# Attention stage: softmax sums after the value products, one reciprocal a head, maxima placed before them

## What is computed

```
mask = q_bucket[:, :, :, None] == k_bucket[:, :, None, :]     # hash of 6 sign bits of q @ proj, k @ proj
scores = scale * np.matmul(q, k.transpose(0, 1, 3, 2))
scores = np.where(mask, scores, -1e9)
scores = scores - np.max(scores, axis=-1, keepdims=True)
attn = np.exp(scores)
attn = attn / (np.sum(attn, axis=-1, keepdims=True) + 1e-09)
attn_out = np.matmul(attn, v)
```

## Time and profile before

| | us |
|---|---|
| median of 3 runs | 670.48 |
| lowest and highest | 669.12, 671.76 |
| the profiled execution | 669.12 |
| its span | 667.0 |

### The profile page before, as it was taken

How to read it: one execution, slowest core, us unless ns; L and a number is a source line. 1 busy time by engine, 2 the same in 40 slices (tenths; PEclk the granted TensorE clock), 3 DMA queues, 4 the chain that set the end, 5 groups by cost and what they waited for, 6 DMA issues and landing times.

```text
span 667.0 us, 9761 instructions
## 1 busy us (share of the span) xinstructions
PE 584.1 (88%) x2886; PEld 437.3 (66%) x2887; DVE 402.7 (60%) x557; ACT 258.7 (39%) x403; POOL 268.8 (40%) x188
## 2 busy tenths in 40 slices
PE   3889999999999979999999996108999999999994
PEld 1566556556566447888888874007887878788773
DVE  3659888888899546556656662724266455556511
ACT  1255454546554522222222243124255364464410
POOL 4378879888887832322332235530000000100101
PEclk9999999999999998999999997558999999999997
DMA  6789578696571011000000003277146645755400
GB/s 188 168 227 242 155 212 213 158 261 171 124 199 29 12 59 68 1 1 0 0 0 0 0 1 126 91 258 259 56 167 209 240 159 179 270 163 180 151 4 30
DMA packets 39266, 83.90 MB, mean 126 GB/s; under 512 B 7485, under 2 KB 10429, under 8 KB 39232
## 3 DMA queue, kind: packets, MB, share of 16 engines
q1 hardware_dynamic: 31376, 71.04, 36.0%
q10 hardware_dynamic: 5616, 6.12, 3.6%
q0 software_dynamic: 2240, 6.31, 2.4%
HBM read 52.09 MB, written 12.35 MB: 97 GB/s over the span
## 4 chain that ended last, share of the span: by engine, by line
PE 75%; ACT 5%; issue 5%; DVE 4%; DMA 4%; POOL 3%; SPq 2%; ACTq 2%; DVEq 0%; POOLq 0%
PE PS L504 9%; PE PS L492 5%; PE PS L662 5%; PE PS L664 4%; PE PS L663 4%; PE PS L472 4%; PE PS L493 4%; PE PS L535 4%; PE PS L643 3%; PE PS L537 3%; PE PS L536 3%; PE PS L644 3%; PE PS L645 3%; PE PS L576 3%; PE PS L578 3%
## 5 line engine op out<-in xcount | busy, mean ns | idle before, releaser
L1033 ACT ACTIVATE at_PT<-PS 128x384 f32<-128x384 f32 x192 | 84.5, 491 | 100.5 <-PE PS L493 99.8
L1248 POOL TENSOR_TENSOR at_acc<-at_acc,at_PT 128x768 f32<-128x768 f32 x64 | 108.0, 1687 | 8.7 <-ACT at_PT L1033 2.8
L958 DVE TENSOR_TENSOR at_W<-at_raw,at_W 128x2048 f32 (+1 forms) x30 | 67.8, 2289 | 70.8 <-ACT at_W L1103 68.2
L728 DVE TENSOR_REDUCE sb_nm<-PS 128x1 f32<-128x768 f32 x96 | 90.2, 955 | 23.1 <-PE PS L472 18.5
L1324 POOL DMA_INDIRECT out<-at_yb,sb_to x16 | 15.8, 986 | 204.9 <-DVE at_yb L970 204.9
L1103 ACT ACTIVATE at_W<-at_raw 128x2048 f32 (+1 forms) x32 | 60.2, 1910 | 60.3 <-issue 34.5
L492 PE MATMUL PS<-at_A,at_B 102*128 102x384 f32 x192 | 75.1, 391 | 7.6 <-ACT at_PT L1033 7.6
L504 PE MATMUL PS<-at_PT,at_V 128*64 128x385 f32 x384 | 68.4, 489 | 2.4 <-ACT at_PT L1033 2.4
L493 PE MATMUL PS<-at_A,at_B 128*128 128x384 f32 x192 | 66.9, 349 | 0.0
L1279 POOL TENSOR_TENSOR at_cn<-at_eb,sb_mv 128x1024 f32<-128x1024 f32 x12 | 22.7, 1896 | 108.0 <-DVE sb_mv L784 108.0
L472 PE MATMUL PS<-at_B,at_A 76*128 76x384 f32 x192 | 57.9, 390 | 6.7 <-DMA at_B<-at_HB 4.7
(11 more groups left out here) (154 smaller groups left out, 1099.5 us busy)
## 6 DMA issues: line engine op xcount, KB each, us to landing
at_raw<-w SPq DMA_DIRECT2D x32, 1024.0 KB, 5.4
at_A<-at_H SPq DMA_DIRECT2D x32, 192.0 KB, 2.7
at_B<-at_H SPq DMA_DIRECT2D x28, 192.0 KB, 3.7
rows_by_expert<-at_empty SPq DMA_DIRECT2D x19, 257.0 KB, 5.3
at_XS<-rows_by_expert ACTq DMA_DIRECT2D x17, 256.0 KB, 2.7
at_stg<-w_solu SPq DMA_DIRECT2D x16, 256.0 KB, 4.1
at_V<-vP SPq DMA_DIRECT2D x16, 192.0 KB, 3.9
at_Re<-qT SPq DMA_DIRECT2D x4, 384.0 KB, 5.0
```

What stands on the lines that cost most here:

```text
L728: dve.tensor_reduce(nm[:, col:col + 1], slot(h, j), AX.XY, ALU.max, negate=True).then_inc(s_nm, 1)
L1033: fn(PT[:, kt, g, 0:HALF], PS[:, STB + g, 0:HALF], ACT.Exp, scale=SCALE).then_inc(s_exp, 1)
L1248: pool.tensor_tensor(total, PT[:, 0, :, 0:HALF] if kt == 1 else total, PT[:, kt, :, 0:HALF], ALU.add).then_inc(s_acc, 1)
```

## The change

PE's order at kt = 2 becomes `turn_maxima(h+1)`, `values(h-1, (3,4,5))`, `sums(h-1)` (before: sums, values, turn). The turn waits for `s_rec` (bank RB read by the sums of two heads before) and for `s_bits`; the sums wait for `s_mc` (the maxima placed), since they share bank RB. At the end `values(15)` stands ahead of `sums(15)`. On DVE `place_maxima(h+1)` moves ahead of the work on head h - 1; the three reciprocals of 128 columns become one of 384, directly behind the denominators; the copy of the epsilon column (L759) moves ahead of them; and `maximum(h+2, 1)` comes behind the whole reciprocal. The wait of `attended` on `s_pv` goes, since `s_rb` now implies it. SP's `load_v(h)` waits for `s_rb >= h - 1`, the sums of head h - 2, in place of `s_pv`. The counts of `s_rec` change from six to three a head.

```diff
@@ -388,7 +388,7 @@
                     fill_2(sp, h, n)
 
             def load_v(h):
-                wait(sp, s_pv, 2 * h - 2)
+                wait(sp, s_rb, h - 1)
                 sp.dma_start(V[h % 2], vP[h:h + 1].rearrange("o p (k d) -> p (o k) d", k=KT)).then_inc(ld_v[h % 2], 16)
 
             def load_w(m):
@@ -475,7 +475,6 @@
 
             def turn_maxima(h):
                 pe.wait_ge(s_mm, h + 1)
-                wait(pe, s_rec, 6 * (h - 1) - 5)
                 m = pe.transpose(PS[0:TILES, RB, 0:P], mm_[:, h % 2 * TILES:(h % 2 + 1) * TILES], ident)
                 m.then_inc(s_mt, 1)
 
@@ -508,8 +507,7 @@
             def sums(h):
 
                 pe.wait_ge(s_acc, (KT - 1) * (h + 1))
-                pe.wait_ge(s_bits, min(PAIRS, 2 + h // 2 + 1))
-                pe.wait_ge(s_mc, min(HEADS, h + 2))
+                wait(pe, s_rec, 3 * h - 1)
                 for g in range(2):
                     m = mm(PS[g * D:(g + 1) * D, RB, 0:HALF], cst[:, C_ONE:C_ONE + D],
                            acc[h % 2][:, g * HALF:(g + 1) * HALF], start=True, stop=True)
@@ -545,18 +543,22 @@
                         leading(*ahead)
                     products(h, kt)
                     if kt == 2:
+                        if h + 1 < HEADS:
+                            wait(pe, s_rec, 3 * h - 4)
+                            pe.wait_ge(s_bits, min(PAIRS, 2 + (h + 1) // 2))
+                            turn_maxima(h + 1)
                         if h > 0:
+                            values(h - 1, (3, 4, 5))
+                            if h + 1 < HEADS:
+                                pe.wait_ge(s_mc, h + 2)
                             sums(h - 1)
-                            values(h - 1, (3, 4, 5))
-                        if h + 1 < HEADS:
-                            turn_maxima(h + 1)
                 values(h, (0, 1, 2))
                 if h % 2 == 0 and h // 2 + 2 < PAIRS:
-                    pe.wait_ge(s_mc, h + 2)
+                    wait(pe, s_rec, 3 * h - 1)
                     hashes(h // 2 + 2, RB)
             hidden(0, 0, 0, True)
+            values(HEADS - 1, (3, 4, 5))
             sums(HEADS - 1)
-            values(HEADS - 1, (3, 4, 5))
             hidden(0, 0, 1, True)
 
 
@@ -743,27 +745,24 @@
                                   ident[0:TILES, 0:TILES].unsqueeze(2).broadcast_to([TILES, TILES, P]),
                                   ALU.mult).then_inc(s_mc, 1)
 
-            def sums_out(h):
+            def inverse(h):
+
                 dve.wait_ge(s_rb, h + 1)
+                dve.tensor_copy(mu[:, h % 2:h % 2 + 1], PS[:, PVB, HALF:HALF + 1]).then_inc(s_rec, 1)
                 dve.tensor_scalar(rec, PS[:, RB, 0:HALF], EPS, None, ALU.add).then_inc(s_rec, 1)
-
-            def inverse(h, n):
-
-                dve.wait_ge(s_rec, 6 * h + 1)
-                dve.reciprocal(rec[:, n * P:(n + 1) * P], rec[:, n * P:(n + 1) * P]).then_inc(s_rec, 1)
+                dve.wait_ge(s_rec, 3 * h + 2)
+                dve.reciprocal(rec, rec).then_inc(s_rec, 1)
 
             def attended(h):
 
                 p, c = h // 2, h % 2
-                dve.wait_ge(s_pv, 2 * h + 2)
-                dve.tensor_copy(mu[:, c:c + 1], PS[:, PVB, HALF:HALF + 1]).then_inc(s_rec, 1)
-                dve.wait_ge(s_rec, 6 * h + 5)
+                dve.wait_ge(s_rec, 3 * h + 3)
                 for g in range(2):
                     mine = slice(g * D, (g + 1) * D)
                     m = dve.scalar_tensor_tensor(
                         out=xT[c * D:(c + 1) * D, p * S + g * HALF:p * S + (g + 1) * HALF], in0=PS[mine, PVB, 0:HALF],
                         scalar=mu[mine, c:c + 1], in1=rec[mine, :], op0=ALU.add, op1=ALU.mult)
-                    m.then_inc(s_rec if g == 0 else s_fin, 1)
+                m.then_inc(s_fin, 1)
 
             def soft(n, b, first):
                 h2 = PS[:, 2 * b:2 * b + 2, :]
@@ -809,23 +808,18 @@
                     hash_bits(h // 2 + 2, RB)
                 if h + 2 < HEADS:
                     maximum(h + 2, 0)
+                if h + 1 < HEADS:
+                    place_maxima(h + 1)
                 if h > 0:
-                    sums_out(h - 1)
-                    inverse(h - 1, 0)
-                    inverse(h - 1, 1)
+                    inverse(h - 1)
                 if h + 2 < HEADS:
                     maximum(h + 2, 1)
                 if h > 0:
-                    inverse(h - 1, 2)
                     attended(h - 1)
-                if h + 1 < HEADS:
-                    place_maxima(h + 1)
                 if h + 2 < HEADS:
                     maximum(h + 2, 2)
                     maximum(h + 2, 3)
-            sums_out(HEADS - 1)
-            for n in range(3):
-                inverse(HEADS - 1, n)
+            inverse(HEADS - 1)
             attended(HEADS - 1)
             soft(0, 0, True)
 
```

## The result

The changed kernel takes 713.26 us in the median of 4 runs (712.05 to 714.27), the kernel before 670.26 in the same comparison. Over all 15 of its runs on record the changed kernel lies between 705.62 and 714.27, with a median of 710.96; the ratio of 1.0609 (95% interval 1.0567 to 1.0651) belongs to these 15, while the two medians of 4 would give 1.064. I had forecast 702.0 (690 to 709). The direction was right, the size too small by 9 to 11 us. The profiled execution of the changed kernel took 709.7 us; its span is 707.6 against 667.0. Nearly all of the 40.6 lies in attention: DVE's L771, the first instruction behind it, starts at 286.71, where it started at 246.43, 40.3 later.

What follows compares the result with a forecast made beforehand. PE taken as the bound, with DVE's chain from sums to values without slack; 30.0 + 1.94 + 1.94 - 0.5 - 0.5 - 0.4 = +32.5 us on 669.1 gives 701.6; predicted 702.0, range 690 to 709.

Steps and rivals of the forecast that it cites:

- DVE's chain without slack: From the end of sums to values(8), DVE's chain takes 5.82 us and PE's work there arrives together with it.
- Sums come 2.14 later: At kt = 2, turn (0.20) and values (1.94) ahead of sums make their end 2.14 us later in each head.
- T to values 5.84: T is the end of sums at kt = 2; in the changed kernel the next values start 5.84 us after it.
- leading(h+2, 3) ends last, by 0.2: On PE, its wait for maximum(h+2,1), 2.3 us, rather than the wait for s_fin, sets when values start, by 0.2.
- No new wait in turn, hashes, SP: The new waits of turn and hashes on PE, and of SP's V loads, would cost nothing.
- Tail: Passes 14 and 15 give back 0.5 us each, values ahead add 1.94 twice, the last chain gives back 0.4.
- The clock: Rival, 5%: PE's 2.3 us pause in every head drops its clock, adding 32 us, for 734 us.
- The rival's price: Loss at the low clock behind each of 14 pauses: 11 matmuls x 0.21 = 2.3 us.
- its sign, L472 at double length behind the pause: Sign of the falling clock: L472 on PE behind the pause runs at double length for more than one instruction.

Runs made afterwards that it cites:

- chain_longer: Kernel before with one more unused reduction ahead of maximum(h+2,1) on DVE in the passes of heads 1 to 13; 683.07 us, ratio 1.0193.
- one_reciprocal: Kernel before with one reciprocal of 384 columns for three of 128, maximum(h+2,1) behind it, PE's order kept; 668.06 us, ratio 0.9948.
- maximum_between: Changed kernel with three reciprocals of 128 columns again and maximum(h+2,1) between the second and third; 703.94 us, ratio 1.0488.
- pause_filled: Changed kernel with 12 small unused matmuls ahead of leading(h+2,3) in the passes of heads 1 to 13; 699.84 us, ratio 1.0436.
- pause_half: Changed kernel with 5 small unused matmuls ahead of leading(h+2,3) in the passes of heads 1 to 13; 706.74 us, ratio 1.054.

## Why the prediction fell short

**DVE's chain without slack: right.** In chain_longer a head grows by the whole 0.87 that was added. The profile's name for the releaser, ACT, was wrong, and the working from the code's own wait was right.

**Sums come 2.14 later: right.** In the chain of waits of the changed kernel, same pass:

```profile
158.84 0.11 PE PS L478
158.95 2.09 PE PS L503 x12
161.04 0.67 PE PS L512 x4
```

These three are 2.87 us, where the sums alone were 0.80: +2.07.

**T to values 5.84: too long.** It is 167.18 - 161.68 = 5.50. The gap of 0.13 ahead of the maximum was PE's doing and vanished, the maximum itself is 0.90 and not 0.96, PE restarts 0.05 behind it and not 0.15, and the copy takes 0.08 of the chain and not 0.14. The reciprocal was priced right: its row is 2.55 long, but the maximum starts 164.86 - 162.39 = 2.47 behind its start. A head at full clock grows by 1.62 to 1.71 (14.08 against 12.46, 15.99 against 14.28) and not by 2.14; 12 of them by 20.0.

**leading(h+2, 3) ends last, by 0.2: wrong, by a little.** In the rows above the products behind it end at 167.13 and L762 at 167.03; PE starts at 167.18. That is 0.15 behind L762, the same 0.15 as behind L763 before (146.11 and 146.26). And it is 0.38 behind the start of the last product (166.80), where one_reciprocal, in which PE has no wait there, needs 0.27 (94.23 to 94.50). So `s_fin` ended last, by some 0.1, and the two waits are nearly a tie. maximum_between shows that freeing the one leaves the other. For the sum it made no difference.

**No new wait in turn, hashes, SP: right.** L743 ends at 159.97, the sums start a us later; the sums, turn and V loads show no wait of their own in the pass.

**Tail: right.** The values in heads 14 and 15 wait 1.35 us for L762, and both passes give some back; L771 starts 286.71 - 282.14 = 4.57 behind the last sums, forecast 4.5. From the sums in pass 14 to L771 the tail grew by 2.46 (30.90 against 28.44), forecast 1.94 + 1.94 - 0.5 - 0.5 - 0.4 = 2.48.

**The clock: this is the step that failed.** I had it as a rival at 5%, all or nothing: "2.3 is nearer 1.68, hence a small chance". The sum put the clock at nothing, and so came out at 702. The pause came out even shorter than I had it, 1.64, and seven of 13 were followed by the low level: 9.7 us in the 12 periods (six of the seven, 1.6 each), some 11 over all by pause_filled. The order alone would have stayed in my range (pause_filled takes 699.84); the clock took the kernel out of it. The rival's price was also off: 2.3 us for each pause, where 1.6 were measured. And its sign, L472 at double length behind the pause, showed only in part: in heads 7 and 11 the pair of L472 took 0.79 and 0.91 us in place of 0.62, but in the pass of head 8, as shown above, L472 and four products ran at full speed, and the slow stretch began with the values, 1.37 us behind the restart. Two errors were in it. I read one event as a rule: the single pause of 1.68 stood alone in a stretch that was otherwise full, and it said nothing of the same pause in every head. And I let the rival be whole or absent, when it could come in part of the heads. Half of its 32 us on top of my sum would have given 718 with my 32.5, 715 with the 29 by which pause_filled is above the kernel before; both are above the 711 to 713 measured. The Trainium skill ("TensorE: Matmul & The Clock Gate", "HAM oscillation") warned of just such a loop; the runs show it at pauses shorter than those it names, 1.64 us in the changed kernel and 1.13 in pause_half.

What adds up, in the two profiled executions:

| stretch | before | changed | more | forecast |
|---|---|---|---|---|
| start to the first sums | 46.90 | 51.78 | 4.9 | 2.1 |
| to the sums in pass 2 | 12.46 | 15.74 | 3.3 | 2.1 |
| 12 periods | 158.63 | 188.29 | 29.7 | 25.7 |
| sums in pass 14 to L771 (L772) | 28.44 | 30.90 | 2.5 | 2.5 |

Together 40.3, where my terms gave 32.4. In the second and third row pause_filled parts the order (1.6 and 20.0) from the clock (1.7 and 9.7). So the order was forecast some 6 too high there, and the clock put back 11.4. The start has one more slow stretch: ahead of the first sums PE waits 3.69 us for ACT, where it waited 1.68 before, and the values behind take 3.78 us and not 2.16. That pause varies from kernel to kernel (4.18 in one_reciprocal, 2.26 in pause_filled), so I put the 2.7 us beyond the forecast on neither the order nor the clock of the loop.

Open: which pauses are followed by the low level. It came in seven of 13 heads behind 1.64 and in seven of 13 behind 1.13, in four of five odd heads behind 1.04 where 0.88 stood close ahead, and in three of 13 behind 0.85 and 0.91 two us apart. It did not come behind 0.34, behind 0.95 or 1.08 alone, or behind 0.75 and 0.95 nearly five us apart. Heads with the same instructions differ (15.99 and 17.65 above), and six heads are slow both at 1.64 and at 1.13. Each count is of one profiled execution, and no run here separates a pause's length from where it falls.

## What to carry to other kernels

When an instruction A starts a long chain on another engine, and PE has work W that nobody waits for, A must come first: W under the chain is free as long as the chain is the longer one, W ahead of it costs nearly its whole length (1.66 of 1.94 us a head here). Before moving it, add up the chain from A to the wait that closes it and compare with PE's work in between; here the chain was the longer by 0.2 us, so that nearly every us moved had to show. A wait that returns in each turn of a loop must be priced with the clock in it, in part of the turns, even where one such wait elsewhere in the trace did no harm.

## What the runs showed of the hardware that I had not expected

- Pauses of PE of 1.64 or 1.13 us, repeated every 14 to 18 us, are followed by stretches at the low clock level in about half of the turns (seven of 13 each), worth 1.6 us each. Small matmuls of no use in the pause (12 of 128 columns) make the kernel some 11 us faster, 9.7 of them in the 12 periods.
- A reciprocal of 128 x 384 takes 2.55 us, one of 128 x 128 0.93: (2553 - 927) / 256 = 6.4 ns a column.
- A wait for two semaphores was put down to ACT in the profile (0.19); chain_longer makes it grow to 0.95, and there it is put down to DVE's L763, whose chain was lengthened.
